# A fused attention, gating unit and mixer: the residual by fp32 transposes of whole y, and another order of masks and loads in the first steps

## The reference

```python
def _attn_ref(q, k, v, n_sink, window):               # 2 x 8 heads x 768 x 64
    keep = is_sink | in_window                        # key < n_sink, or 0 <= query - key < window
    scores = np.where(keep, scale * q @ k.T, -1e9)
    ...                                               # softmax over the keys, then @ v
def _moe_ref(x, w_in, w_spatial, b_spatial, w_out):   # x: (2, 768, 512)
    h = np.maximum(x @ w_in, 0.0)                     # 1024 columns: u and v
    v_n = (v - mu) / np.sqrt(var + 1e-06)
    v_s = np.einsum('ts,bsd->btd', w_spatial, v_n) + b_spatial[None, :, None]
    return (u * v_s) @ w_out                          # y
def _moe2_ref(x, w_tok1, w_tok2, w_ch1, w_ch2):       # x is y
    h = np.maximum(x.transpose(0, 2, 1) @ w_tok1, 0.0) @ w_tok2
    u = x + h.transpose(0, 2, 1)
    return u + np.maximum(u @ w_ch1, 0.0) @ w_ch2
```

## Time and profile before

| | |
|---|---|
| median of 3 runs | 522.99 us (522.36 to 523.8) |
| the profiled execution | 523.14 us, of which the span from first to last instruction is 521.4 |
| granted PE clock in the records | 1.00 |
| busy: PE, DVE, ACT, POOL | 498.1, 217.3, 151.7, 178.5 us |

### The profile page before, as it was taken

One profiled execution on the slowest core, in us unless ns is written; L12 is line 12 of the kernel. 1 busy time (PEld: TensorE's weight loads), 2 busy tenths in 40 slices (PEclk: granted clock), 3 DMA queues, 4 the chain that ended last, 5 costly groups with the idle time before them and its releaser, 6 DMA issues.

```text
span 521.4 us, 7223 instructions
## 1 busy us (share of the span) xinstructions
PE 498.1 (96%) x2712; PEld 442.9 (85%) x2712; DVE 217.3 (42%) x535; ACT 151.7 (29%) x315; POOL 178.5 (34%) x192
## 2 busy tenths in 40 slices
PE   2589999999999999999999999999999999999997
PEld 1578899999999989999888899888888888888885
DVE  4577777587567434755221232112121121211212
ACT  3246656466555342111221122110101101001010
POOL 5566645375343278900406912950000000000000
PEclk9999999999999999999999999999999999999999
DMA  7524332433220134300201410410001000010002
GB/s 264 163 89 156 104 96 77 126 119 105 84 82 0 47 121 127 92 15 1 75 1 61 137 47 6 136 40 1 0 19 63 0 1 0 18 64 1 0 1 80
DMA packets 19478, 34.18 MB, mean 66 GB/s; under 512 B 2288, under 2 KB 4848, under 8 KB 19440
## 3 DMA queue, kind: packets, MB, share of 16 engines
q1 hardware_dynamic: 19008, 33.55, 20.3%
q10 hardware_dynamic: 432, 0.13, 0.1%
HBM read 30.53 MB, written 3.15 MB: 65 GB/s over the span
## 4 chain that ended last, share of the span: by engine, by line
PE 89%; DVE 4%; issue 2%; DMA 1%; POOL 1%; ACT 1%; DVEq 0%; ACTq 0%; SPq 0%
PE bank L933 23%; PE bank L935 23%; PE bank L934 23%; PE bank L1006 7%; PE bank L972 3%; PE bank L948 2%; PE bank L949 2%; PE bank L1014 1%; PE bank L988 1%; PE bank L1166 1%; DVE q_st L751 1%; DMA mask_scratch<-key 1%; PE bank L1164 1%; DVE masked L760 1%; DMA stage<-w_sp 1%
## 5 line engine op out<-in xcount | busy, mean ns | idle before, releaser
L922 DVE SCALAR_TENSOR_TENSOR hch_lo<-bank,hch_hi 128x512 fp32r<-128x512 f32 x36 | 24.9, 692 | 153.8 <-ACT hch_hi L696 153.8
L696 ACT ACTIVATE hch_hi<-bank 128x512 fp32r<-128x512 f32 x36 | 21.5, 598 | 169.0 <-PE bank L935 169.0
L588 ACT ACTIVATE probs<-masked,small 128x288 f32<-128x288 f32 (+1 forms) x96 | 49.1, 512 | 64.4 <-DVE small L760 64.2
L760 DVE CUSTOM_DVE_ANT_0 masked<-bank,masks 128x288 f32<-128x288 f32 (+1 forms) x96 | 40.9, 427 | 38.4 <-PE bank L949 32.7
L935 PE MATMUL bank<-up_hi,wc_lo 128*128 128x512 f32 x144 | 56.0, 389 | 0.0
L934 PE MATMUL bank<-up_lo,wc_hi 128*128 128x512 f32 x144 | 56.0, 389 | 0.0
L933 PE MATMUL bank<-hch_hi,wc_hi 128*128 128x512 f32 x144 | 56.0, 389 | 0.0
L934 PE MATMUL bank<-hch_lo,wc_hi 128*128 128x512 f32 x144 | 56.0, 389 | 0.0
L933 PE MATMUL bank<-up_hi,wc_hi 128*128 128x512 f32 x144 | 56.0, 389 | 0.0
L935 PE MATMUL bank<-hch_hi,wc_lo 128*128 128x512 f32 x144 | 56.0, 389 | 0.0
L948 PE MATMUL bank<-k_hi,q_st 128*128 128x288 f32 (+1 forms) x96 | 35.5, 372 | 18.2 <-DVE q_st L751 12.8
(11 more groups left out here) (120 smaller groups left out, 1067.2 us busy)
## 6 DMA issues: line engine op xcount, KB each, us to landing
k_raw<-kT SPq DMA_DIRECT2D x24, 256.0 KB, 3.1
q_raw<-qT SPq DMA_DIRECT2D x24, 256.0 KB, 2.7
stage<-w_c SPq DMA_DIRECT2D x24, 256.0 KB, 2.6
v_sl<-vL SPq DMA_DIRECT2D x12, 264.0 KB, 2.8
outT<-out_sb SPq DMA_DIRECT2D x12, 256.0 KB, 2.1
stage<-w_sp SPq DMA_DIRECT2D x12, 192.0 KB, 2.5
stage<-w_in SPq DMA_DIRECT2D x8, 256.0 KB, 3.6
stage<-w_out SPq DMA_DIRECT2D x4, 256.0 KB, 3.2
```

The costliest lines, as they stand in the source:

```text
L588: act.activation(probs[:, n % N_PROB, 0:w], masked[:, n % N_MASKED, 0:w], ACT.Exp, bias=least[:, n % 8:n % 8 + 1], scale=-1.0).then_inc(ex ...
L696: act.activation(hch_hi[:, u[2] % N_HCH, :], bank[:, :], ACT.Relu).then_inc(hi_ready, 1)
L760: dve.tensor_tensor_reduce(masked[:, n % N_MASKED, 0:w], score_bank[n % 2][:, 0:w], masks[:, m:m + w], 1.0, 3e38, ALU.add, ALU.min, least[ ...
L922: dve.scalar_tensor_tensor(out=hch_lo[:, f % N_HCH, :], in0=bank[:, :], scalar=0.0, in1=hch_hi[:, f % N_HCH, :], op0=ALU.max, op1=ALU.subt ...
```

## The change

It has five parts.

- Residual: ACT writes, beside `y_hi`, a whole fp32 copy of each y tile (`y_f`, one more activation a unit). PE brings y in by three fp32 transposes a unit (`is_transpose=True`, `ident`) in place of six fp32r matmuls. `identr` goes. DVE's `y_lo` waits for the copy, and ACT's first copy waits until all `g_lo` are written.
- Since `y_f` lies where parts of wc1 are to go, wc1's second third waits for p's first half, and its last third for all of p, behind `wc2_0` to `wc2_2`.
- POOL makes the position tables by two `iota`; ACT's queue loads `params` alone. DVE's first comparison comes before its wait for `params`.
- ACT writes the second, even and odd masks (at steps 2, 9 and 17) by `mask_by_act`; DVE makes only `prev_keep` and `second_keep`, at step 1, and `general_flag` moves from step 0 to 2. ACT also writes the high parts of the eight `w_in` pieces; POOL keeps the low parts.
- SP issues k and q of group 2 ahead of the three `w_in` pieces, v of tile 1 behind them, the sinks' values later, behind the fifth piece. POOL's `sinks_prepare(0)` moves from step 1 to 3.

```diff
+        y_f = [[at(f"y_f0_{s}", D_Y_F + DM * s if s < NT // 2 else A_WC1 + CH * (s - NT // 2) + 512, [DM])
+                for s in range(NT)],
+               [at(f"y_f1_{s}", A_WC1 + CH * s + 2 * 512, [DM]) for s in range(NT)]]
...
+        channel_up_pieces(0, PH_Y)
+        channel_up_pieces(1, (ready, index[("p", 0, 1, KT - 1)] + 1))
+        channel_down_pieces(0, 3)
+        channel_up_pieces(2, PH_P)
+        channel_down_pieces(3, NF)
...
+                    if g == 3:
+                        load_sink_values(0)
...
             load_qk(0)
             load_qk(1)
             load_v(0)
-            load_sinks(0)
-            load_v(1)
+            load_sink_keys(0)
+            load_qk(2)
             for n in range(3):
                 stage_in(n)
-            load_qk(2)
+            load_v(1)
...
+            pool.iota(rel_sb, [[-1, P]], base=0, channel_multiplier=1, allow_small_or_imprecise_dtypes=True).then_inc(s_const, 1)
+            pool.iota(key_sb, [[1, P]], base=0, channel_multiplier=0, allow_small_or_imprecise_dtypes=True).then_inc(s_const, 1)
...
-                if n == 1:
+                if n == 3:
                     sinks_prepare(0)
...
                 if n % 4 == 2 and n // 4 < EARLY:
-                    split_weight(n // 4)
+                    low_weight(n // 4)
...
+            def mask_by_act(*parts):
+                act.wait_ge(keeps_ready, 1)
+                for at_, keep, w in parts:
+                    ins = act.activation(masks[:, at_:at_ + w], keep[:, 0:w], ACT.Copy, bias=MASKED, scale=-MASKED)
+                ins.then_inc(later_masks, 1)
...
             act.dma_start(par_i[:, :], params).then_inc(s_par, 16)
-            act.dma_start(rel_sb, rel[:, 0:P]).then_inc(s_const, 16)
-            act.dma_start(key_sb, key[:, 0:P]).then_inc(s_const, 16)
...
+                if n == 2:
+                    mask_by_act((MASK_SECOND, second_keep, P), (MASK_SECOND + P + SINKS, diag_keep, P))
+                if n == 9:
+                    mask_by_act((MASK_EVEN, diag_keep, P), (MASK_EVEN + P, sink_keep, SINKS), (MASK_EVEN + P + SINKS, prev_keep, P))
+                if n == 17:
+                    mask_by_act((MASK_ODD, prev_keep, P), (MASK_ODD + P, sink_keep, SINKS), (MASK_ODD + P + SINKS, diag_keep, P))
...
+                if n % 4 == 2 and n // 4 < EARLY:
+                    weight_high(n // 4)
...
                 if u[0] == "y":
+                    if u[1:] == (0, 0):
+                        act.wait_ge(g_lo_ready, 2 * B * KT)
                     act.activation(y_hi[u[1]][:, u[2], :], bank[:, :], ACT.Copy).then_inc(hi_ready, 1)
+                    act.activation(y_f[u[1]][u[2]][:, :], bank[:, :], ACT.Copy).then_inc(y_f_ready, 1)
...
             def first_mask():
+                dve.wait_ge(s_const, 2)
+                done(dve.tensor_scalar(diag_keep, rel_sb, 0.0, None, ALU.is_ge))
                 dve.wait_ge(s_par, 16)
...
-            def second_mask():
+            def later_keeps():
                 done(dve.tensor_scalar(prev_keep, rel_sb, float(P), par[:, 1:2], ALU.add, ALU.is_lt))
-                done(dve.tensor_tensor(second_keep, prev_keep, sink_keep, ALU.max))
                 dve.memset(masks[:, MASK_SECOND + P:MASK_SECOND + P + SINKS], MASKED)
...
+                dve.tensor_tensor(second_keep, prev_keep, sink_keep, ALU.max).then_inc(keeps_ready, 1)
...
+                if h == 0 and 1 <= t <= 3:
+                    dve.wait_ge(later_masks, t)
...
-                if n == 0:
+                if n == 1:
+                    later_keeps()
+                if n == 2:
                     general_flag()
...
                 if u[0] == "y":
+                    dve.wait_ge(y_f_ready, NT * u[1] + u[2] + 1)
...
+                    if d == 0:
+                        pe.wait_ge(y_f_ready, NT * b + NT // 2 * (c + 1))
                     for m in range(NT // 2):
-                        s = NT // 2 * c + m
-                        pe.matmul(out[:, P * m:P * m + P], y_hi[b][:, s, own], identr[:, :], start=m == 0, stop=False,
-                                  skip_group_check=True)
-                        pe.matmul(out[:, P * m:P * m + P], y_lo[b][:, s, own], identr[:, :], start=False, stop=False,
-                                  skip_group_check=True)
+                        pe.matmul(out[:, P * m:P * m + P], y_f[b][NT // 2 * c + m][:, own], ident[:, :], start=m == 0, stop=False,
+                                  is_transpose=True, skip_group_check=True)
```

More of the change, by code:

```diff
@@ L174 @@
 E_ID = E_STAGE + 3 * 512
-E_IDR = E_ID + P
-COLS = E_IDR + P
+COLS = E_ID + P
 assert all(at % P == 0 for at in (A_V, A_PROBS, A_PT, A_PTS, A_CAT, A_X, B_X, X_SLOT, B_WIN, C_VN, D_U, E_V, E_STAGE, E_ID))
@@ L188 @@
 C_WC2 = C_VN
+D_Y_F = D_U + 2 * B * (TOK // P) * DM + (TOK // P) * S
 D_HT = D_U
@@ L194 @@
 assert 2 * KT * CH <= A_WT1
-assert B_WT2_HI + (TOK // P) * S <= C_VN and D_WT2_LO + (TOK // P) * S <= E_V and D_OUT + KT * CHUNK <= E_V
+assert B_WT2_HI + (TOK // P) * S <= C_VN and D_Y_F + NT // 2 * DM <= E_V + 2 * FH and D_OUT + KT * CHUNK <= E_V
 def build(nc, qT, kT, kS, vL, vS_in, w_in, w_sp, b_sp, w_out, w_t1, w_t2, w_c1, w_c2, rel, key, params,
@@ L238, in build @@
         ident = at("ident", E_ID, [P])
-        identr = at("identr", E_IDR, [P], F32R)
         small = at("small", E_SMALL, [80])
@@ L364, in build, with channel_up_pieces, channel_down_pieces @@
                 piece("wt2", wt2_hi[:, k:k + 1, cols], wt2_lo[:, k:k + 1, cols], w_t2[:, k:k + 1, cols], PH_G)
-        for c in range(CH // 512):
+        def channel_up_pieces(c, phase):
+            cols = slice(512 * c, 512 * c + 512)
             for k in range(KT):
-                cols = slice(512 * c, 512 * c + 512)
-                piece(f"wc1_{c}", wc1_hi[:, k:k + 1, cols], wc1_lo[:, k:k + 1, cols], w_c1[:, k:k + 1, cols], PH_Y)
-        for f in range(NF):
-            piece(f"wc2_{f}", wc2_hi[:, f:f + 1, :], wc2_lo[:, f:f + 1, :], w_c2[:, f:f + 1, :], PH_P)
+                piece(f"wc1_{c}", wc1_hi[:, k:k + 1, cols], wc1_lo[:, k:k + 1, cols], w_c1[:, k:k + 1, cols], phase)
+        def channel_down_pieces(first, last):
+            for f in range(first, last):
+                piece(f"wc2_{f}", wc2_hi[:, f:f + 1, :], wc2_lo[:, f:f + 1, :], w_c2[:, f:f + 1, :], PH_P)
+        channel_up_pieces(0, PH_Y)
[3 more added lines that the diff above has]
+        channel_down_pieces(3, NF)
         def staged(n):
@@ L399, in load_v, with load_sink_keys @@
                 sp.dma_start(v_sl[:, t % 3, :], vL[t]).then_inc(s_v[t % 3], 16)
-            def load_sinks(b):
+            def load_sink_keys(b):
                 if b:
@@ L428, in attention_loads @@
                         stage_in(g + 1)
+                    if g == 3:
+                        load_sink_values(0)
                     if g == 2 * NT + 3:
-                        load_sinks(1)
+                        load_sink_keys(1)
+                        load_sink_values(1)
                     if is_general and g % 2 and g < 2 * TILES + 3:
@@ L713, in first_mask @@
                 done(dve.tensor_copy(par_f[:, 1:4:2], par_i[:, 1:4:2].bitcast(I32)))
-                dve.scalar_tensor_tensor(out=par, in0=par_f[:, 1:4:2], scalar=4294967296.0, in1=par_f[:, 0:4:2],
-                                         op0=ALU.mult, op1=ALU.add).then_inc(s_mask, 1)
-                dve.wait_ge(s_const, 32)
-                dve.tensor_scalar(diag_keep, rel_sb, 0.0, None, ALU.is_ge).then_inc(s_mask, 1)
-                steps[0] += 2
-                dve.wait_ge(s_mask, steps[0])
+                done(dve.scalar_tensor_tensor(out=par, in0=par_f[:, 1:4:2], scalar=4294967296.0, in1=par_f[:, 0:4:2],
+                                              op0=ALU.mult, op1=ALU.add))
                 dve.tensor_scalar(sink_keep, key_sb, par[:, 0:1], None, ALU.is_lt)
@@ L730, in general_flag @@
                 dve.tensor_copy(general[:, :], fits[:, 2:3]).then_inc(s_general, 1)
-            def second_mask():
+            def later_keeps():
                 done(dve.tensor_scalar(prev_keep, rel_sb, float(P), par[:, 1:2], ALU.add, ALU.is_lt))
-                done(dve.tensor_tensor(second_keep, prev_keep, sink_keep, ALU.max))
                 dve.memset(masks[:, MASK_SECOND + P:MASK_SECOND + P + SINKS], MASKED)
-                to_mask(MASK_SECOND, second_keep, P)
-                done(to_mask(MASK_SECOND + P + SINKS, diag_keep, P))
-            def even_mask():
-                to_mask(MASK_EVEN, diag_keep, P)
-                to_mask(MASK_EVEN + P, sink_keep, SINKS)
-                done(to_mask(MASK_EVEN + P + SINKS, prev_keep, P))
-            def odd_mask():
-                to_mask(MASK_ODD, prev_keep, P)
-                to_mask(MASK_ODD + P, sink_keep, SINKS)
-                done(to_mask(MASK_ODD + P + SINKS, diag_keep, P))
+                dve.tensor_tensor(second_keep, prev_keep, sink_keep, ALU.max).then_inc(keeps_ready, 1)
             def q_low(g):
@@ L1071, in _ @@
```

(2 more changed lines are left out.)

18 lines of the change are left out of this document (6 added, 12 removed).

## The result

The changed kernel takes **509.93 us** (median of 6 runs, 509.34 to 510.43), against 522.99 (521.07 to 524.14) for the kernel before, measured beside it: a ratio of 0.975 [0.973, 0.977], 13.1 us faster. The forecast was 513.7, from 511.0 to 517.7. The direction was right, the size was not: the gain lies 3.8 us above the forecast and 1.1 us beyond the range. The profiled execution took 509.37 us, with a span of 507.5.

A forecast was written before the change was run, and what follows sets the result against it. PE, busy 96% of the span, bounds the kernel, except in the head, where DVE and first loads rule. Stage p 5.3 plus head 4.0 (4.5 - 0.5) gives 9.3 us: 513.7 us, range 511.0 to 517.7.

The forecast's parts named there:

- Stage p: Residual rebuild, 16 units: three fp32 transposes replace six identity matmuls, saving 0.33 us each, 5.3 us (4.5 to 5.8).
- The 12 copies of y by ACT: ACT's extra fp32 copies of y fit its idle time and cost nothing; without that cover, 7.2 us.
- POOL's weight pieces: Reordered wc1 and wc2 pieces are ready before PE wants them, four from the middle of p; no new stall.
- rival d: The clock falls in stage p because of the transposes, 22.4 us more, 536 us; chance 0.03.
- The first score: Start of the kernel: first score at 7.6 us in place of 10.14, 2.5 us earlier (2.3 to 3.1).
- From there to the branch: First score to general-flag branch: DVE sheds masks, net 2.4 us (1.4 to 3.0), of which 2.0 let through.
- rival a: Head gives nothing lasting: late w_in pieces hold ACT, whose extra 7 us replace DVE's; 517.7 us; chance beyond 516.5: 0.13.
- The pause of 3.66 I leave as it is: DVE's 3.66 us issue pause behind the general-flag branch stays, since nothing in the change takes the branch away.
- Relief from POOL: DVE's gain from less overlap with POOL, left out of the sum and kept for the range.
- the head: 0 to 38 us, where DVE and the first loads rule: gain 4.0 us, between 1.5 and 6.5.
- The even mask at step 9: ACT's even mask stands ahead of q_high(3), which DVE and PE await: 0.8 us, of which 0.5 charged.
- rival b: PE reaches its full clock 3 us sooner; with POOL's relief the head gives 7 us: 510.7 us; chance 0.11.

The follow-up runs named there:

- e1: The kernel before with the residual part of the change alone (whole y, fp32 transposes, weight-piece order); 515.96 us, ratio 0.988.
- e2: The changed kernel with the old residual (fp32r identity matmuls), so the head part alone; 515.22 us, ratio 0.986.
- e7: The changed kernel with the old order of loads (w_in before k and q of group 2, sinks early); 509.38 us, ratio 0.973.
- e13: The changed kernel with a DVE wait for its own last instruction ahead of reading the flag; 509.76 us, ratio 0.976.
- e14: The kernel before with the wait that ends the odd mask moved behind the branch; 521.55 us, ratio 0.998.
- e9: The kernel before with SP holding loads from q of group 4 on until the ninth masked score; 522.70 us, ratio 0.999.
- e15: e6 with SP's loads from the fifth w_in piece on held until DVE masked the first score behind the branch; 513.43 us, ratio 0.981.
- e6: The changed kernel with the second, even and odd masks made by DVE again; 514.38 us, ratio 0.983.
- e8: The changed kernel with the high halves of the eight w_in pieces on POOL again; 511.41 us, ratio 0.976.
- e10: The changed kernel with 8 more DVE instructions in the skipped general path; 509.56 us, ratio 0.974.
- e16: The changed kernel with k and q of group 3 issued ahead of SP's wait for the flag; 509.46 us, ratio 0.975.
- e12: The changed kernel with DVE reading the flag at step 6, branch still at step 8; 509.65 us, ratio 0.974.
- e5: The changed kernel with the position tables loaded by ACT's queue again in place of the two iotas; 511.17 us, ratio 0.976.
- e3: The kernel before without the branch on the general flag and without the general path; 516.74 us, ratio 0.990.
- e4: The changed kernel without the branch on the general flag and without the general path; 507.67 us, ratio 0.972.

## Why the prediction fell short

**Stage p was right.** Forecast 5.3 us (4.5 to 5.8): the units went from 1.73 to 1.38, 16 x 0.35 = 5.6, 5.5 between the milestones and 5.9 by e1's median. The rows for the transposes of probs priced it. The 12 copies of y by ACT were hidden, as argued: from stage s to stage p it is 99.0 us in both kernels. POOL's weight pieces came as worked out:

```profile
297.40 0.62 POOL L532 TENSOR_SCALAR wc_hi<-stage 128x512 fp32r<-128x512 f32 x1 [19.56 <-PE bank L952]
...
308.48 0.62 POOL L532 TENSOR_SCALAR wc_hi<-stage 128x512 fp32r<-128x512 f32 x1 [3.20 <-PE bank L952]
```

That is the timeline of POOL in the kernel after: four pieces from the middle of p, the next ones from its end at 308.2, and PE waits for none in stage h.

**The clock in stage p did not fall** (rival d). The 48 transposes took 270 to 273 ns each, and the six matmuls of a unit took 287.35 - 286.21 = 1.14 us (1.12 in before). The rule of the Trainium skill that the full clock doesn't engage for transposes ("TensorE: Matmul & The Clock Gate", Part 4: PE-mode transpose) does not hold for transposes that stand among matmuls here.

**The first score: nearly right.** Forecast 7.6 (q_low from 6.3, ending between 7.0 and 7.7), measured 7.14. Each step up to 6.3 came out within 0.15 us: parameters, three short steps, the operation beside k_lo (ends at 5.46, forecast 5.6), mask done at 6.31 (forecast 6.3). Only the last choice was wrong: q_low at 6.35 stood ahead of POOL's second k_lo (7.17), so it took 0.69. That is 0.5 us, and it hangs on which comes first: in e2 and e7, with POOL first, the score came at 8.14 and 8.07.

**From there to the branch.** Forecast 2.0 us more, of a range of 1.4 to 3.0, measured 2.5. The first w_in piece landed at 11.3 (forecast 10.9) and ACT did wait 1.15 us for it, ahead of its fourth exponential (rival a); e7, which loads these pieces earlier, was no faster, so this wait cost nothing that can be measured. POOL finished k_prepare(2) at 16.77 (forecast 16.2) and did come last before step 8, which the forecast had named as a sign of its failing: PE's step 8 began 0.1 us behind it. That too cost nothing, because DVE could not have taken the score before 19.23.

**The step that failed is "The pause of 3.66 I leave as it is".** DVE's stop went from 4.78 to 3.26 us. The forecast took the pause alone for the stop and a constant; its row has 0.97 us of reading ahead of it. By giving the masks to ACT the change also takes away the wait that kept this reading behind DVE's last instruction (e13: +0.87 us of stop; e14: some 0.7 of its 1.3), and it brings the branch to a time when SP issues no loads (0.7 in e9, 1.1 in e15; here the 0.6 that is left). Together 1.5 us. Put as parts of the change: the masks on ACT are worth 4 to 5 us (e6), of which 2.2 is DVE's earlier arrival and 1.8 the stop; the forecast had 2.0 for the first and 0 for the second.

**Relief from POOL: left out of the sum.** "What DVE gains by less overlap with POOL I leave out" was 0.7 to 1.8 us for the w_in pieces (e8), with intervals that overlap. In the first pair of profiles steps 10 to 16 went in 9.25 us in place of 10.91, but this 1.66 isn't shown to be a gain: the same steps took 8.8 to 10.9 us in the four kernels with the head and branch of before (before, e1, e9 and e14; mean 9.8), and 8.8 to 10.8 in six with those of after (after, e10 to e13 and e16; mean 9.5).

**The even mask at step 9** was charged 0.5 us. It does delay q_high(3) by that much (DVE's q_low waits 0.93 us for it in after, 0.41 in e6), but PE was at its transposes and value matmuls meanwhile and started the next score at 23.20 with no idle time. It cost nothing in this profile.

**PE's clock** rose sooner than said (rival b). Timeline of PE, kernel after, four transposes of probs and the value matmuls between:

```profile
24.35 1.05 PE L989 MATMUL bank<-ident,probs 128*128 128x128 f32 x4
25.19 1.22 PE L1023 MATMUL bank<-v_sl,p_t 128*128 128x66 f32 x8
...
27.22 0.60 PE L989 MATMUL bank<-ident,probs 128*128 128x128 f32 x4
```

The level changed within the eight value matmuls at 25.19 (1.22 us, where the same eight take 1.00 us at 27.65); in before it changed at about 33.7. That is 8 us sooner, and the stop ended 7.0 sooner; one us less at half the clock is worth 0.5 by the forecast's own reckoning. The forecast had 29. The moment itself scatters: in e12, whose stop ended at 19.00, PE's score matmuls were still slow at 27.90 (0.44 us, in after 0.29 at 26.95) and the level changed within the value matmuls at 29.23, some 4 us later than in after. That is part of why e12 took 10.8 us for steps 10 to 16.

**The count.** At the end of the stop the kernel after was 7.0 us ahead, where the forecast had 4.5: first score 0.5, way to the branch 0.5, stop 1.5. With the 0.5 that the even mask was charged and didn't cost, that makes 7.0 for the head against 4.0, between the 6.6 of e2 and the 7.6 of the medians; the further 1.3 us of the first pair of profiles came in steps 10 to 16 and is scatter as far as the runs tell. Stage p adds 0.2 to 0.6. So half of what the forecast missed in the head is the stop, and the first score's part is luck of the order. What stays open: how the values of e5 and e7 would add up (their differences lie within the intervals), and why 1.8 us pass between the instruction packet and DVE's next instruction.

## What to carry to other kernels

Read a stop as the whole idle time of the engine, from its last instruction to its next, and ask for each piece of it what has to come first: a wait on the engine's own last instruction ahead of a read and a branch puts the read into the stop. When a change takes work from an engine in front of such a place, look at what waited for that work, and which transfers are issued then; neither is a constant. Before a difference between two profiles is called a gain, look at the same stretch in other kernels that share it. And when PE's operand is already in SBUF in fp32, three fp32 transposes in place of six fp32r matmuls with an identity can be a saving; here the rows of other transposes of the same shape priced it beforehand.

## What the runs showed of the hardware

- Behind a taken branch DVE paused 2.95 us (e9) and 2.86 us (e15) with no load issued in the 5 us ahead of it, 3.07 (e14) with one issued 1.0 us ahead, and 3.66 and 3.60 (before, e1) with two issued in the last 1.3 us. 8 or 64 more instructions to jump over changed the stop by 0.05 us at most. One packet of the instruction queue q14 came 1.8 to 1.9 us before the end of each of these pauses, and e3 and e4, without the branch, have none between 14 and 22 us.
- Reading the flag from memory into a register and comparing took 0.96 to 0.97 us on DVE (before, e9, e15). In e14, with no wait between, it began while DVE's mask instructions were still under way.
- Of a DVE instruction and a POOL k_lo that started together, one went at its own pace and the other took longer: q_low 0.69 alone and 1.80 behind a k_lo of 1.26, k_lo 1.83 behind q_low, a 128x128 TENSOR_SCALAR 1.34 beside k_lo where another took 0.23. DVE's 128x128 mask instruction, which reads the scores from PSUM, took 0.29 both beside k_lo (15.67 in after) and without it (7.83).
- An iota of 128x128 in fp32 took 0.24 us on POOL (after).
- 48 fp32 transposes of 128x128 among full matmuls took 270 to 273 ns each, three of them 0.24 us from the first to the next matmul, where six fp32r matmuls with an identity took 0.61 (after, before).
